# Linear attention with two MLP blocks: token mixing per pair of heads inside the attention loop, states and their products in 64-row and 64-column form

## The reference

```python
# attention, per head, in blocks of positions, written here for one block
intra = (q k^T * decay_mask) v
inter = (q * lam^(i+1)) state
state = lam^block * state + (k * lam^(block-1-i))^T v
# token mixing, x is [2, 768, 512]
h = relu(x^T @ w_tok1) @ w_tok2          # 768 -> 256 -> 768 over the positions
u = x + h^T
u = u + relu(u @ w_ch1) @ w_ch2          # first MLP, 512 -> 1536 -> 512
u = u + real(fft over positions and channels)
u = u + relu(layernorm(u) @ w_ch1b) @ w_ch2b    # second MLP, 512 -> 2048 -> 512
```

## Time and profile before

| | us |
|---|---|
| median of the three runs (630.82, 634.16, 632.91) | 632.91 |
| span of the profiled execution, first to last instruction | 631.7 |
| start of the scores of head 1 in it | 15.81 |
| end of attention, start of token mixing | 82.45 |
| start of the first `up` | 118.81 |

### The profile page before, as it was taken

How to read it: one execution, slowest core, us unless ns; L and a number is a source line. 1 busy time by engine, 2 the same in 40 slices (tenths; PEclk the granted TensorE clock), 3 DMA queues, 4 the chain that set the end, 5 groups by cost and what they waited for, 6 DMA issues and landing times.

```text
span 631.7 us, 8134 instructions
## 1 busy us (share of the span) xinstructions
PE 615.2 (97%) x3332; PEld 551.8 (87%) x3332; DVE 297.8 (47%) x547; ACT 170.8 (27%) x277; POOL 67.0 (11%) x120
## 2 busy tenths in 40 slices
PE   6799899999999999999999999999999999999997
PEld 3798888989999888988898888989889999988886
DVE  5979745624343276234465832446532522222223
ACT  2125212323242223222233322222322222222220
POOL 6886000030000010000000100000000000000000
PEclk9879989999999999999999999999999999999999
DMA  8536132032132112020211211120222221122302
GB/s 313 194 110 228 65 101 66 1 105 66 67 103 79 57 67 67 35 66 35 67 42 59 68 35 65 34 66 34 67 66 68 67 66 55 48 66 67 133 1 100
DMA packets 24564, 49.01 MB, mean 78 GB/s; under 512 B 3020, under 2 KB 3920, under 8 KB 24528
## 3 DMA queue, kind: packets, MB, share of 16 engines
q1 hardware_dynamic: 23520, 45.90, 22.4%
q0 software_dynamic: 576, 1.72, 0.9%
q10 hardware_dynamic: 432, 0.88, 0.4%
HBM read 45.35 MB, written 3.15 MB: 77 GB/s over the span
## 4 chain that ended last, share of the span: by engine, by line
PE 91%; DVE 5%; DMA 3%; issue 1%; ACT 0%; SPq 0%; ACTq 0%; DVEq 0%
PE banks L770 28%; PE banks L771 28%; PE banks L772 28%; DMA vns<-vn_dram 2%; PE banks L819 2%; PE banks L825 2%; DVE state L552 1%; PE banks L815 1%; PE banks L779 1%; DVE pt L535 1%; DVE qdec L514 1%; DVE u L622 1%; PE banks L791 0%; DMA lamb<-lam_dram 0%; DVE dpad L475 0%
## 5 line engine op out<-in xcount | busy, mean ns | idle before, releaser
L770 PE MATMUL banks<-uth,wl 128*128 128x384 f32 x448 | 150.7, 336 | 0.0
L772 PE MATMUL banks<-uth,wh 128*128 128x384 f32 x448 | 150.6, 336 | 0.0
L771 PE MATMUL banks<-utl,wh 128*128 128x384 f32 x448 | 150.4, 336 | 0.0
L770 PE MATMUL banks<-wh,hl 128*128 128x512 f32 x336 | 134.4, 400 | 0.0
L771 PE MATMUL banks<-wl,hh 128*128 128x512 f32 x336 | 133.1, 396 | 0.0
L772 PE MATMUL banks<-wh,hh 128*128 128x512 f32 x336 | 132.8, 395 | 0.0
L455 DVE TENSOR_TENSOR wl<-raw,wh 128x1024 fp32r<-128x1024 f32 x56 | 68.4, 1223 | 132.1 <-ACT wh L318 132.0
L581 DVE SCALAR_TENSOR_TENSOR hl<-banks,hh 128x384 fp32r<-128x384 f32 x112 | 61.9, 556 | 92.4 <-ACT hh L422 92.3
L318 ACT ACTIVATE wh<-raw 128x1024 fp32r<-128x1024 f32 x56 | 59.2, 1059 | 145.4 <-PE banks L772 145.3
L422 ACT ACTIVATE hh<-banks 128x384 fp32r<-128x384 f32 x112 | 54.8, 491 | 141.1 <-PE banks L772 141.1
L770 PEld LDWEIGHTS banks<-uth,wl 128*128 128x128 f32 x448 | 84.2, 188 | 2.5
(11 more groups left out here) (152 smaller groups left out, 545.9 us busy)
## 6 DMA issues: line engine op xcount, KB each, us to landing
raw<-w1b_dram SPq DMA_DIRECT2D x32, 256.0 KB, 2.7
raw<-w2b_dram SPq DMA_DIRECT2D x32, 256.0 KB, 2.9
raw<-w1a_dram SPq DMA_DIRECT2D x24, 256.0 KB, 2.7
raw<-w2a_dram SPq DMA_DIRECT2D x24, 256.0 KB, 2.9
kTs<-kT_dram SPq DMA_DIRECT2D x8, 384.0 KB, 3.2
qTs<-qT_dram SPq DMA_DIRECT2D x8, 384.0 KB, 3.9
out_dram<-u SPq DMA_DIRECT2D x12, 256.0 KB, 2.6
kns<-kn_dram SPq DMA_DIRECT2D x7, 384.0 KB, 5.0
```

What stands on the lines that cost most here:

```text
L770: mm(o, ll, rh_, start=start, stop=False)
L771: mm(o, lh, rl_, start=False, stop=False)
L772: return mm(o, lh, rh_, start=False, stop=stop)
```

## The change

- Each head's attention result no longer goes to full-width xh and xl (two batches x 6 tiles x 512 channels) but to a buffer of one pair of heads (128 channels x 2 batches). Token mixing is done per pair of heads p: `tokmix1` (36 products of 256 columns), `tokmix2` (36), and `mixed_transposes` (12). All this for pairs 0 to 2 stands in PE's list between the products of the next two heads; that of pair 3 follows the last head.
- The transposes of both batches are done there; `SIDE_FIRST` is gone.
- `state` is [128, 2, 5, 64] instead of block diagonal. State products are ten of 64 columns (batch 0 in the left, batch 1 in the right column half), the q-state products ten of 64 rows. The state chain on DVE is five operations of 128x64 instead of ten of 64x64.
- Scores use two banks instead of four, so each half of a head's scores waits for the mask of the half before it.
- k is decayed in place. `place_x` on ACT makes xh, waits for xl, then copies the result into u, with two small copies per batch for edge rows, which had been six DVE additions after attention.
- POOL builds the masks of heads 1 to 7; t1l is made on DVE instead of POOL; the first k and v loads are issued before ACT waits for `lam`.
- `weights_hi/lo` of steps 0 and 1 stand in the lists of ACT and DVE at the end of heads 4 and 5.
- The products of `up` step 0 are spread around the token mixing of pair 3 (`up_part`).

```diff
-        att, ring = ExitStack(), ExitStack()
-        xh = sb(att, "xh", [L, 2 * NC, DM], f32r)
+        xh = sb(att, "xh", [L, B, NC, L], f32r)
...
-        state = sb(ring, "state", [L, 2, NC - 1, L])
+        state = sb(att, "state", [L, 2, NC - 1, D])
...
-            for h in range(2, H):
+            for h in range(1, H):
...
             def decay_k(h):
...
                 act.wait_ge(s_kv[h % NI], loaded(h))
-                if h >= 2:
-                    act.wait_ge(kv_done, h - 1)
-                copy(kdec[:, h % 2, :, :], kns[:, h % NI, :, :], scale=lrev[:, h:h + 1]).then_inc(kdec_ready, 1)
+                copy(kns[:, h % NI, :, :], kns[:, h % NI, :, :], scale=lrev[:, h:h + 1]).then_inc(kdec_ready, 1)
+            def place_x(h):
...
+                for b in range(B):
+                    act.wait_ge(att_done, 2 * h + b + 1)
...
+                    copy(xh[:, b, :, half], o).then_inc(xh_ready, 1)
+                for b in range(B):
+                    act.wait_ge(xl_ready, 2 * h + b + 1)
...
+                    copy(u[:, NC * b:NC * (b + 1), chans], o).then_inc(x_copied, 1)
+                    act.wait_ge(x_copied, 2 * h + b + 1)
+                    copy(u[0:1, NC * b + NA:NC * b + NA + 1, chans], o[0:1, NC - 1:NC, :])
+                    copy(u[0:1, NC * b + NA + 1:NC * (b + 1), chans], o[0:1, NA:NC - 1, :]).then_inc(x_placed, 1)
...
             for h in range(H):
+                if h >= 2 and h % 2 == 0:
+                    g_hi(h // 2 - 1)
+                if h >= 3 and h % 2:
+                    mixed_hi(h // 2 - 1, 0)
                 if h + 2 < H:
                     decay_k(h + 2)
...
+                if h == 1:
...
+                    copy(t1h[:, :, :], t1raw[:, :, :]).then_inc(t1h_ready, 1)
+                place_x(h)
+                if h >= 3 and h % 2:
+                    mixed_hi(h // 2 - 1, 1)
+                    mixed_hi(h // 2 - 1, 2)
+                if h == 1:
+                    copy(t2h[:, :, :], t2raw[:, :, :]).then_inc(t2h_ready, 1)
+                if h in (4, 5):
+                    weights_hi(h - 4)
...
+            for h in range(H):
                 if h + 1 < H:
+                    mask(h + 1, 0)
...
+                elif h % 2 == 0:
+                    states(h + 1)
+                    mask(h + 1, 1)
                     decay_q(h + 1)
+                    g_lo(h // 2 - 1)
...
+                else:
+                    mix_added(h // 2 - 1, 0)
+                    mask(h + 1, 1)
+                    states(h + 1)
+                    mix_added(h // 2 - 1, 1)
+                    mixed_lo(h // 2 - 1, 0)
+                    decay_q(h + 1)
+                    mix_added(h // 2 - 1, 2)
+                x_lo(h)
+                if h >= 3 and h % 2:
+                    mixed_lo(h // 2 - 1, 1)
+                    mixed_lo(h // 2 - 1, 2)
+                if h in (4, 5):
+                    weights_lo(h - 4)
...
+                    for b in range(B):
+                        rows = slice(D * b, D * (b + 1))
+                        last = mm(bank[2][rows, c * D:(c + 1) * D], kns[:, h % NI, c, rows], vns[:, h % NI, c, rows],
+                                  start=True, stop=True, skip_group_check=True)
...
+            def scores(h, half):
...
+                if h or half:
+                    pe.wait_ge(mask_done, 2 * h + half)
...
+            for h in range(H):
...
+                if h + 1 < H:
+                    scores(h + 1, 0)
+                if h < 2:
+                    scores(h + 1, 1)
+                    state_products(h + 1)
+                    attend(h)
+                elif h % 2 == 0:
+                    state_products(h + 1)
+                    tokmix1(p, 0)
+                    scores(h + 1, 1)
+                    tokmix1(p, 1)
+                    attend(h)
+                else:
+                    tokmix2(p, 0)
+                    if h + 1 < H:
+                        scores(h + 1, 1)
+                        state_products(h + 1)
+                    tokmix2(p, 1)
+                    mixed_transposes(p, 0)
+                    tokmix2(p, 2)
+                    attend(h)
+                    mixed_transposes(p, 1)
+                    mixed_transposes(p, 2)
+            p = NP - 1
...
+            pe.wait_ge(utl_ready, 3 * p)
...
+            up_part(0, 0, KD - 1)
+            tokmix1(p, 0)
+            tokmix1(p, 1)
+            pe.wait_ge(x_placed, 2 * H)
+            up_part(1, 0, KD - 1)
...
+            for half in range(2):
+                pe.wait_ge(utl_ready, 3 * p + half + 2)
+                up_part(half, KD - 1, KD).then_inc(h_done, 1)
```

More of the change, by code:

```diff
@@ L796, in _ @@
-            pe.wait_ge(warm_ready, 1)
-            for i in range(WARM):
-                last = mm(bank[7][:, :], state[:, 0, 0, :], state[:, 0, 1:, :], start=True, stop=True)
-            last.then_inc(warm_done, 1)
-            scores(0)
-            state_products(0)
-            for h in range(H):
-                if h + 1 < H:
-                    scores(h + 1)
-                    state_products(h + 1)
+                if h or half:
+                    pe.wait_ge(mask_done, 2 * h + half)
@@ new lines, in attend @@
+                if h:
+                    pe.wait_ge(xl_ready, 2 * h)
+                    pe.wait_ge(x_placed, 2 * h)
+                for c in range(1, NC):
+                    for b in range(B):
+                        rows, cols = slice(D * b, D * (b + 1)), slice(slot(c) * D, (slot(c) + 1) * D)
+                        mm(bank[6 + b][:, cols], qdec[rows, h % 2, c, :], state[rows, h % 2, c - 1, :],
+                           start=(c == 1), stop=True, skip_group_check=True)
+                pe.wait_ge(mask_done, 2 * h + 2)
@@ L821, in _ @@
+                for b in range(B):
+                    for c in range(NC):
+                        last = mm(bank[6 + b][:, slot(c) * D:(slot(c) + 1) * D], pt[:, h % 2, b, c, :],
+                                  vns[:, h % NI, c, D * b:D * (b + 1)], start=False, stop=True, skip_group_check=True)
                     last.then_inc(att_done, 1)
@@ new lines, in tokmix1 @@
+            def tokmix1(p, m):
+                if m == 0:
+                    pe.wait_ge(t1l_ready, 1)
+                    pe.wait_ge(xl_ready, 4 * (p + 1))
+                    tokmix_bank_read(p, 0)
+                o = tokmix_bank(p, 0)[:, m * B * L:(m + 1) * B * L]
+                cols = slice(m * L, (m + 1) * L)
+                for t in range(NC):
+                    c = slot(t)
+                    last = mm3(o, t1h[:, c, cols], t1l[:, c, cols], xh[:, :, t, :], xl[:, :, t, :], t == 0, t == NC - 1)
+                if m == KT - 1:
+                    last.then_inc(g_done, 1)
@@ new lines, in up_part @@
+            def up_part(half, k0, k1):
+                cols = slice(half * HALF, (half + 1) * HALF)
+                for k in range(k0, k1):
+                    kc = slice(k * L, (k + 1) * L)
+                    last = mm3(bank[6 + half][:, 0:HALF], wh[0][:, 0, kc], wl[0][:, 0, kc],
+                               uth[:, 0, k, cols], utl[:, 0, k, cols], k == 0, k == KD - 1)
+                return last
+            pe.wait_ge(warm_ready, 1)
+            for i in range(WARM):
+                last = mm(bank[7][:, :], pt[:, 0, 0, 0, :], pt[:, 0, 0, 1:5, :], start=True, stop=True)
```

410 lines of the change are left out of this document (200 added, 210 removed).

## The result

| | before | after |
|---|---|---|
| median, us (four runs each) | 632.4 | 654.66 (650.66 to 656.12) |
| span of the profiled execution | 631.7 | 648.8 |
| end of the attention products of head 7 | 82.45 | 122.0 |
| end of the first `up` | 123.0 | 142.2 |

A forecast was written before the change was run, and what follows sets the result against it. PE (TensorE), 91% of the chain, was taken as the bound. The first `up` ends 19.6 us later, less 2.6 for transposes: +17.0 on the 631.7 span, 648.7, plus 1.2 for the median: 649.9 us, range 634 to 658.

The forecast's parts named there:

- the long stall: Before head 6's second half scores, PE idles 8.7 us: its mask stands behind step 0's wl, which awaits a late load.
- The 1.6 at head 6: PE waits 1.6 us at head 6 because step 1's wh and wl stand before the mask of head 7.
- the 3.8 at the tail: After head 7's attention PE idles 3.8 us before `up_part`, which waits for the last utl of pair 2.
- E0: End of head 0's attention products, forecast at 26.5 us (23.4 at full clock).
- E1: End of head 1's attention products, forecast 8.3 us after head 0's, at 34.8 us.
- so I take half clock until 24: At the start, after little PE work, the clock was assumed at half until 24 us: 3.2 us of work done, 5.7 wanted.
- the sum: Added PE work in attention: 2.2 us for narrower token mixing plus 3.8 for tile-shape changes, 6.0; state products stay at 1.1.
- The 0.29 taken: Price in us of one tile-shape excursion among full products; ten more excursions and 12 inner changes made +3.8 us.
- D: Rival: step 0's weight load arrives in time and the clock holds; same time, 635.3 us; chance 0.13.
- A: Rival: new work fills PE's holes; faster, 621 us at best, about 627 with waits; chance 0.12.
- B: Rival: shape changes are free and the clock stays at 1.00; slower by less, 640.2 us; chance 0.19.
- C: Rival: more half clock, behind waits before `up_part` and at heads 2 and 6; slower by more, 656.3 us; chance 0.12.

The follow-up runs named there:

- experiment 1: Changed kernel with weights of steps 0 and 1 made at the end of heads 6 and 7 instead of 4 and 5; 646.2 us, ratio 1.0226.
- experiment 2: Changed kernel with SP issuing the weight loads of steps 0 to 2 ahead of head 7's load; 650.7 us.
- experiment 11: Changed kernel with rows of unused products of several shapes behind the last down, run for their durations alone; an excursion with 64 rows takes 0.37 us.
- experiment 6: Changed kernel with step 0 weights after head 7, step 1 weights behind pair 3's hidden, first `up` part behind its tokmix1, and unused products early; 630.66 us, ratio 0.9965.
- experiment 10: Kernel before with 25 unused products in its three idle places (heads 0, 2 and 7); 625.97 us, ratio 0.9895.
- experiment 3: As experiment 1, with the first part of `up` and its waits moved behind tokmix1 of pair 3; 642.4 us, ratio 1.0156.
- experiment 7: The kernel of experiment 6 without its unused products; 638.8 us, ratio 1.0081.

## Why the prediction was right

Slower, by 3.3% where 2.7% were forecast, and the long stall is where and what it was said to be. Point by point, forecast and trace of after in us:

| end of attention of head | 0 | 1 | 2 | 3 | 4 | 5 | 6 | 7 | first `up` |
|---|---|---|---|---|---|---|---|---|---|
| forecast | 26.5 | 34.8 | 48.1 | 60.6 | 73.5 | 97.5 | 112.0 | 121.1 | 142.6 |
| measured | 29.4 | 39.5 | 51.3 | 62.9 | 75.2 | 99.5 | 113.2 | 122.0 | 142.2 |

- **The long stall** was priced at 8.7 us and is 9.92, since the load takes 9.1 us and not 7.9; the 2.8 us of half clock behind it are 3.1. Experiments 1 and 2 show its parts: the load 7.1, the place in the lists 2.8. The 1.6 at head 6 are 1.44, the 3.8 at the tail 3.10.
- **E0 and E1** were 2.9 and 4.7 us too early. The step that failed is "so I take half clock until 24": it lasted until 35.8, through most of head 1. The kernel before had two stretches there, with full clock in between; with the masks between the halves of the scores PE idles three times, 2.33, 2.56 and 1.25 us, and the clock does not come back in between. A smaller part is POOL's mask of head 1, "ready at 16.5" by a row of 0.45 us: its last two steps take 0.77 and 0.72, and it is over 1.3 us later, at 17.76:

```profile
17.04 0.72 POOL L256 TENSOR_TENSOR dmask<-pwork,dpool 128x128 f32<-128x128 f32 x1
```

The mask is 1.3 of the 2.9 us at E0; the other 1.6, and the 1.8 more at E1, are what the longer half clock leaves over the shorter work of these heads.
- **The later heads** were too long in the walk and gave this error back: 11.8 instead of 13.3 for head 2, 11.6 instead of 12.5 for head 3, 12.3 instead of 12.9 for head 4, 13.7 instead of 14.5 for head 6. Twenty state products take 0.73 us (54.69 to 55.42), not 1.1. By the rule weighed in the prediction (Trainium skill, "TensorEngine Tiling (Array Packing)", Key Properties), that different tiles work in parallel, it would be 0.6; the 0.73 of the trace is nearer to that than to the 1.1 of the sum. The half scores and the state products of head 4, with 0.21 us before and 0.22 behind them, where a product of 256 columns has 0.12, cost 0.19 as an excursion; alone (experiment 11) it is 0.32 to 0.37. The 0.29 taken lies between.
- **A product of 256 columns** has a pitch of 0.12, as taken from 258 columns. The q-state products take 1.26 (1.4), the pt products 2.82 (2.4).
- **The sum.** +6.0 us of PE work net were forecast. The account by the trace of after leaves 3.3, the comparison of experiments 6 and 10 gives 4.3; both are below it.
- **The level.** That the span of the profiled run, 648.8, meets the 648.7 of the walk is luck: its errors of up to 4.7 us cancel. The median is 4.8 us above the forecast since that run is the shortest: the other three have clocks of 0.961 to 0.966 instead of 0.974. 0.010 of 650 us are 6.5 us of lost clock. It may lie in a longer stretch at the start or in one behind the tail's wait, as experiments 1 and 2 show both; those three have no trace that would tell which.
- **The rivals.** D (the load is no wait) is refuted by the 9.06 us. A asked for less than 11.8 us of idle time and half clock; there were 38. B's clock at 1.00 came only with unused products, and the changes of shape are not free (experiment 11). C, more half clock, is in the median: in the profiled run more of it than forecast lies at the start, and none behind the 3.10 and the 1.44 us that C named, but the same 3.10 us have it behind them in experiments 1 and 2.

## What to carry to other kernels

When work is moved into another part of the program, walk it on every queue: the reader of a load may move ahead while the load stays behind others in its queue, and everything listed behind that reader stops. An idle time in front of dense work can cost more by the clock behind it than by itself: in the kernel before, 2.4 us of it at 26.6 to 30.5 had 10.2 us of half clock behind them, 4.9 us lost. Unused products in three such places gave 1.05% there, while the change studied here, which reorders the real work, cost 3.3%. And before reckoning with a change of shape, count how often the shape alternates.

## What was not expected of the hardware

- Half clock at the start lasted 20.5 us in after and 31 to 34 in experiments 1, 2, 3 and 7, which have the same instructions there; one kernel's runs spread over 5 to 10 us by it (641.0 to 651.1 in experiment 2). What ends such a stretch was not settled. Dense attention products did not end it in experiment 1: the second window there is busy for all of its 11.1 us, at 0.50.
- The same idle time of 3.10 us, at the same place, had 1.00 behind it in after and 0.50 in experiment 1. Its length alone does not tell.
- fp32 products of 64 columns in one column half run at 0.058 us each, about half of the full shape's 0.112, though both are 64 columns wide.
- A switch between full products and row or column halves costs 0.32 to 0.37 us there and back in rows of such products (experiment 11) and 0.19 in the running kernel; a switch between fp32 and its rounded form costs nothing.
